# Two units of 576 and four of 720 tokens instead of seven of 576, with a six-place ring carried on from the first unit

## The reference

```python
k_p = k.reshape(B, H, Sp, 8, D).mean(axis=3)      # B = H = 8, D = 64, Sp = 576 // 8 = 72
v_p = v.reshape(B, H, Sp, 8, D).mean(axis=3)
attn = softmax(matmul(q, k_p.transpose(0, 1, 3, 2)) / sqrt(D))
x = matmul(attn, v_p).transpose(0, 2, 1, 3).reshape(4608, 512)
h = x @ moe_w_in;   g = s * relu(h) ** 2 + b;   x = g @ moe_w_out       # layer 0
h = x @ moe2_w_in;  g = h / (1 + exp(-h));      out = g @ moe2_w_out    # layer 1
```

## Time and profile before

| | us |
|---|---|
| three runs | 1695.22, 1687.95, 1694.45 (median 1694.45) |
| the profiled execution's own time | 1693.99 |
| its span, first to last instruction | 1692.2 |
| TensorE / DVE / ACT / GpSimd busy | 1614.3 / 1073.7 / 927.5 / 239.5 |
| mean granted TensorE clock | 0.982 of 2.4 GHz |
| DMA | 542.75 MB, mean 321 GB/s |

### The profile page before, as it was taken

The page is one execution under the profiler, slowest core; times in us unless marked ns, Lnnn a source line. Parts: engine busy times, 40 slices in busy tenths (PEclk is TensorE's granted clock), DMA queues, the critical chain, the costliest instruction groups (busy, mean ns, idle before and its releaser), DMA issues.

```text
span 1692.2 us, 29600 instructions
## 1 busy us (share of the span) xinstructions
PE 1614.3 (95%) x11926; PEld 1600.0 (95%) x11926; DVE 1073.7 (63%) x1309; ACT 927.5 (55%) x1286; POOL 239.5 (14%) x294
## 2 busy tenths in 40 slices
PE   7988997899999999999999999999999999999999
PEld 6988997899999999999999999999999999999998
DVE  6686677376574757557575674837657475654645
ACT  4574554565547555574555645556454755547443
POOL 5320220120201112011120201112011120000000
PEclk9999999999999999999999999999999999999999
DMA  6789787989898998989889898998989899899997
GB/s 191 278 321 346 297 313 291 394 295 326 300 374 306 340 322 301 378 307 332 303 317 376 298 339 306 359 350 299 325 295 384 307 333 316 272 391 330 331 327 259
DMA packets 155222, 542.75 MB, mean 321 GB/s; under 512 B 16592, under 2 KB 16592, under 8 KB 153040
## 3 DMA queue, kind: packets, MB, share of 16 engines
q1 hardware_dynamic: 150736, 531.43, 87.2%
q10 hardware_dynamic: 4352, 9.44, 1.4%
HBM read 464.39 MB, written 76.41 MB: 320 GB/s over the span
## 4 chain that ended last, share of the span: by engine, by line
PE 76%; DMA 10%; DVE 8%; ACT 3%; issue 2%; SPq 0%; DVEq 0%; ACTq 0%
PE a_ps L745 20%; PE a_ps L767 20%; PE b_ps L767 15%; PE b_ps L745 13%; DMA xa_dram<-probs 6%; PE a_ps L671 2%; DMA w_raw<-weights 2%; PE t_ps L625 2%; PE t_ps L638 2%; DMA ring<-w_dram 2%; DVE w_sum L1156 2%; DVE ring L1141 1%; PE t_ps L611 1%; ACT ring L840 1%; DVE gq L1200 1%
## 5 line engine op out<-in xcount | busy, mean ns | idle before, releaser
L745 PE MATMUL a_ps<-xc_hi,ring 128*128 128x288 f32 x1792 | 404.5, 304 | 20.2 <-DVE gq L1200 15.7
L767 PE MATMUL a_ps<-sp_hi,ring 128*128 128x288 f32 x1792 | 368.7, 295 | 1.4 <-DMA ring<-w_dram 1.4
L745 PEld LDWEIGHTS a_ps<-xc_hi,ring 128*128 128x128 f32 x1792 | 306.7, 193 | 24.0 <-DVE gq L1200 17.7
L745 PE MATMUL b_ps<-xc_hi,ring 128*128 128x288 f32 x1344 | 302.4, 300 | 13.7 <-DVE gq L1200 13.6
L767 PEld LDWEIGHTS a_ps<-sp_hi,ring 128*128 128x128 f32 x1792 | 291.2, 188 | 1.9 <-DMA ring<-w_dram 1.9
L1241 DVE TENSOR_TENSOR sp_lo<-gq,sp_hi 128x1152 fp32r<-128x1152 f32 (+1 forms) x182 | 198.1, 1101 | 132.5 <-ACT sp_hi L937 131.7
L767 PE MATMUL b_ps<-sp_hi,ring 128*128 128x288 f32 x1344 | 277.8, 295 | 0.6 <-DMA ring<-w_dram 0.6
L745 PE MATMUL a_ps<-xc_lo,ring 128*128 128x288 f32 x896 | 269.4, 301 | 0.0
L767 PE MATMUL a_ps<-sp_lo,ring 128*128 128x288 f32 x896 | 264.5, 295 | 0.0
L745 PEld LDWEIGHTS b_ps<-xc_hi,ring 128*128 128x128 f32 x1344 | 228.5, 191 | 15.3 <-DVE gq L1200 15.0
L937 ACT ACTIVATE sp_hi<-gq 128x1152 fp32r<-128x1152 f32 (+1 forms) x182 | 168.2, 940 | 126.5 <-PE b_ps L767 63.4
(11 more groups left out here) (168 smaller groups left out, 2570.6 us busy)
## 6 DMA issues: line engine op xcount, KB each, us to landing
ring<-w_dram SPq DMA_DIRECT2D x784, 512.0 KB, 5.6
w_dram<-w_stage SPq DMA_DIRECT2D x32, 1024.0 KB, 6.5
w_dram<-ring SPq DMA_DIRECT2D x48, 512.0 KB, 3.9
w_raw<-weights SPq DMA_DIRECT2D x16, 1024.0 KB, 6.4
out<-yb ACTq DMA_DIRECT2D x16, 576.0 KB, 7.2
k_stage<-kT SPq DMA_DIRECT2D x30, 288.0 KB, 5.7
q_sb<-qT SPq DMA_DIRECT2D x30, 288.0 KB, 6.0
v_stage<-vP SPq DMA_DIRECT2D x30, 288.0 KB
```

Source lines behind the costliest of these rows:

```text
L745: last = nc.tensor.matmul(bank[:, half, 0:th], w, xc_of(x, th)[:, j, k, :], start=(first and k == 0 and i == 0), stop=(k == 1 and i == 2), ...
L767: last = nc.tensor.matmul(bank[:, m, 0:th], w, split_of(g, th, turn, 2 * c + half), start=(first and half == 0 and i == 0), stop=(end and ...
```

## The change

Units have 576, 576, 720, 720, 720 and 720 tokens (`HALVES`). Attention stands six jobs beside each of units 0 and 1 (bases 2, 17, 32, 47, 62, 77), four beside each of units 2, 3 and 4 (0, 17, 56, 71), none beside unit 5; the first unit's third and fourth job begin at 66 and 83. The ring has six places, and granule n of unit 0 on goes to place (64 + n) mod 6, so that the first unit's granules and the next ones follow each other; the first four are asked for at i = 0, 1, 5, 6 of set 15. Split down pieces have four places (still written three pieces ahead). x is loaded into parts of `gq` that are free (behind its first unit's part, or where the third quarter ends), later in the odd phase (behind the low part of down piece 7), and ACT's first copy of an even phase waits until all of x is split. The raw weights, their sums and their stage lie over parts of `yb`, `xc_hi`, `xc_lo`, `sp_hi` and `sp_lo`. In the first unit the second half of a set's split stands at i = 6 instead of i = 2, its stores at 1, 2 and 7, DVE's `plain_out` first in its slot, and x is loaded behind slot 100 and used from 108.

```diff
-HALVES = (288,) * 7
+HALVES = (288,) * 2 + (360,) * 4
...
-XR_SLOTS = (11, 13, 15, 17, 19, 21, 23)
-RING = 8
+XR_SLOTS = (15, 17, 19, 21, 23, 25, 27)
+RING = 6
+PLACES = 4
...
-FIRST_XR = (36, 39, 42, 45, 48, 51, 54)
+LAST_LOADS = (0, 1, 5, 6)
+FIRST_XR = (44, 46, 49, 51, 54, 57, 59)
+XC_FIRST, SP_FIRST, G_FIRST = 14 * HB, 4 * PLACES * HB, 2 * FS * HB
...
+def place_of(n):
+    return (4 * SETS + n) % RING
...
-FIRST_TURNS = ((0, SPACED), (17, SPACED), (64, SPACED), (81, SPACED))
-TURN_SLOTS = ((0, SPACED), (17, OVER_EDGE), (SLOTS, TIGHT), (SLOTS + 15, TIGHT))
+FIRST_UP = 2
+FIRST_TURNS = ((0, SPACED), (17, SPACED), (66, SPACED), (83, SPACED))
+SIX = tuple((2 + 15 * n, TIGHT) for n in range(6))
+FOUR = ((0, SPACED), (17, OVER_EDGE), (SLOTS, TIGHT), (SLOTS + 15, TIGHT))
+UNIT_TURNS = (FIRST_TURNS, SIX, SIX, FOUR, FOUR, FOUR)
...
+        def x_of(ph):
+            s, layer = divmod(ph, 2)
+            if layer:
+                return yb[:, :]
+            at = 24 * HALVES[s - 1] if s else G_FIRST
+            return gq[:, at:at + 2 * KC * HALVES[s]]
...
+        def ring_stored(granule):
+            stored = [n for n in range(granule % RING, granule + 1, RING) if n % 4 != 2]
+            assert granule % 4 != 2
+            return r_stored[granule % RING], len(stored) * DMA
...
@@ load_gran
-                    sp.wait_ge(f_done, (SETS - 2 + n // 4) * PLAIN + PLAIN)
-                    if n % 4 != 2:
-                        sp.wait_ge(r_stored[n], SETS // 2 * DMA)
-                sp.dma_start(ring[:, n % RING, :].bitcast(F32), w_dram[row_of(ph, slot)]
+                    q, m = divmod(4 * SETS + n - RING, 4)
+                    sp.wait_ge(f_done, q * PLAIN + m + 5)
+                    sp.wait_ge(*ring_stored(4 * q + m if m != 2 else 4 * q + m - RING))
+                sp.dma_start(ring[:, place_of(n), :].bitcast(F32), w_dram[row_of(ph, slot)]
@@ load_x
-                    sp.wait_ge(xlo_ready, (2 * s - 1) * NPROD)
+                    sp.wait_ge(dlo_ready, (2 * s - 1) * SPLITS + PIECE_END[7])
@@ SP, first unit
-                if i < 4 and q + 1 < SETS:
-                    store_plain(q + 1, i)
+                if i in (1, 2, 7) and q + 1 < SETS:
+                    store_plain(q + 1, {1: 0, 2: 1, 7: 3}[i])
...
+                if q == SETS - 1 and i in LAST_LOADS:
+                    load_gran(0, LAST_LOADS.index(i))
...
-                if slot == FSLOTS - 30:
+                if slot == FSLOTS - 28:
                     load_x(0)
@@ SP, units
-                    if layer and slot == SLOTS_UP + RING + 3 and s + 1 < UNITS:
+                    if layer and slot == SLOTS_UP + RING + 10 and s + 1 < UNITS:
@@ ACT, prep_plain
-                if q >= 2:
-                    act.wait_ge(f_done, (q - 2) * PLAIN + 6 + 2 * n)
+                old_q, old_n = divmod(2 * q + n - RING // 2, 2)
+                if old_q >= 0:
+                    act.wait_ge(f_done, old_q * PLAIN + 6 + 2 * old_n)
@@ ACT, plain_out, layer 1
+                    act.wait_ge(f_sum, 4 * (SETS - 1))
+                    act.wait_ge(f_wlo, 2 * (SETS - 1))
@@ ACT, dhi
-                old_ph, old_idx = divmod(nth - 3, len(DOWN))
+                old_ph, old_idx = divmod(nth - PLACES, len(DOWN))
@@ ACT, part_up
+                if ph % 2 == 0 and g == 0 and j == 0:
+                    act.wait_ge(xlo_ready, (ph + 1) * NPROD)
@@ ACT and DVE, first unit
-                if i in (0, 2) and q + 1 < SETS:
-                    prep_plain(q + 1, i // 2)
+                if i in (0, 6) and q + 1 < SETS:
+                    prep_plain(q + 1, i // 6)
@@ DVE, first unit: the same two lines moved from the end of the slot to before prep_plain
                 if q % 8 == 7 and i % 2:
                     plain_out(q, i // 2)
```

More of the change, by code:

```diff
@@ L108 @@
 OVER_EDGE = (0, 1, 2, 3, 4, 6, 7, 8, 9, 11, 12, 14, 15)
-FIRST_TURNS = ((0, SPACED), (17, SPACED), (64, SPACED), (81, SPACED))
 TIGHT = (0, 1, 2, 3, 4, 6, 7, 8, 9, 11, 12, 13, 14)
-TURN_SLOTS = ((0, SPACED), (17, OVER_EDGE), (SLOTS, TIGHT), (SLOTS + 15, TIGHT))
+FIRST_UP = 2
[3 more added lines that the diff above has]
+UNIT_TURNS = (FIRST_TURNS, SIX, SIX, FOUR, FOUR, FOUR)
 def schedule():
     table, t = {}, PAIRS
[L117 to L121, removed]
+    for s, slots in enumerate(UNIT_TURNS, -1):
+        for base, offsets in slots:
             for i, name in zip(offsets, TURN_NAMES):
-                table[s, base + i] = (name, job)
-        t = upto
+                assert (s, base + i) not in table
+                table[s, base + i] = (name, t)
+            t += 1
+        assert t >= batches_for(s + 1) * PAIRS
     assert t == JOBS
@@ L217, in build, with over @@
         t_ps = psum("t_ps")
-        x_stage = probs[:, 0:S]
+        def over(name, at, columns, shape, dt=F32):
+            return nc.alloc_sbuf_tensor_at(name, [P] + shape, dt, offset=at + 4 * columns)
+        w_raw = [over("w_raw0", yb_at, 0, [4, 512]), sb("w_raw1", [P, 4, 512])]
+        w_sum = [over("w_sum0", xc_hi_at, XC_FIRST, [2, 512]), over("w_sum1", xc_lo_at, XC_FIRST, [2, 512])]
+        w_stage = [over("w_stage0", sp_hi_at, SP_FIRST, [2, GRAN], F32R), over("w_stage1", sp_lo_at, SP_FIRST, [2, GRAN], F32R)]
+        x_stage = probs[:, 0:S]
+        def x_of(ph):
[4 more added lines that the diff above has]
+            return gq[:, at:at + 2 * KC * HALVES[s]]
         def xc_of(buf, th):
@@ L449, in store_sum @@
                 sp.dma_start(w_dram[row:row + step + 1:step].rearrange("j p n -> p j n"),
-                             w_stage[:, (2 * q + n) % STAGE, :, :].bitcast(F32)).then_inc(done, DMA)
+                             w_stage[(2 * q + n) % STAGE][:, :, :].bitcast(F32)).then_inc(done, DMA)
             def sets_of(ph, slot):
@@ L684, in plain_down @@
                     if k == 3:
-                        pe.wait_ge(x_summed, 4 + 4 * layer)
+                        pe.wait_ge(x_summed, 2 * FIRST_UP * (1 + layer))
                     else:
@@ L751, in down @@
                 idx, c = divmod(slot - SLOTS_UP, 2)
-                (j, h), turn = DOWN[idx], (ph * len(DOWN) + idx) % 3
+                (j, h), turn = DOWN[idx], (ph * len(DOWN) + idx) % PLACES
                 n, th = gran(ph, slot) - 1, HALVES[ph // 2]
@@ L1144, in sum_set @@
             def sum_set(q, n):
-                a11, a12, a21, a22 = [w_raw[:, q % 2, i, :] for i in range(4)]
-                s1, s2 = w_sum[:, 0, :], w_sum[:, 1, :]
+                a11, a12, a21, a22 = [w_raw[q % 2][:, i, :] for i in range(4)]
+                s1, s2 = w_sum[0][:, 0, :], w_sum[0][:, 1, :]
                 if n == 0:
@@ L1155, in sum_set @@
                     left, right = ((s1, a11), (a12, s2), (a11, a21))[n - 1]
-                nc.vector.tensor_tensor(w_sum[:, n, :], left, right, ALU.subtract if n else ALU.add).then_inc(f_sum, 1)
+                nc.vector.tensor_tensor(w_sum[n // 2][:, n % 2, :], left, right, ALU.subtract if n else ALU.add).then_inc(f_sum, 1)
             def low_sum(q, n):
-                done = by_pair(w_stage[:, (2 * q + n) % STAGE, :, :])
+                done = by_pair(w_stage[(2 * q + n) % STAGE][:, :, :])
                 dve.wait_ge(f_whi, sum_split(q, n))
@@ L1350, in _ @@
                 attention(*turn_at(-1, slot))
-                if i in (0, 2) and q + 1 < SETS:
-                    prep_plain(q + 1, i // 2)
+                if q % 8 == 7 and i % 2:
+                    plain_out(q, i // 2)
+                if i in (0, 6) and q + 1 < SETS:
+                    prep_plain(q + 1, i // 6)
                 if i < 4:
@@ L1360, in _ @@
                     x_slot(0, XORDER[FIRST_XR.index(at)])
-                if q % 8 == 7 and i % 2:
-                    plain_out(q, i // 2)
             for ph in range(PHASES):
```

70 lines of the change are left out of this document (36 added, 34 removed).

## The result

The change makes the kernel 0.6% faster, a small gain but outside the interval of the noise: 1681.91 us median (1673.23 to 1686.48, 11 runs) against 1691.85 (1684.14 to 1698.28, 11 runs), ratio 0.9937, 95% interval 0.9912 to 0.9963. The prediction said 1650 with a range from 1608 to 1674: the sign is right, a gain of 42 was foretold and 10 came. The profiled execution took 1683.26 us, its span 1681.5.

What follows compares the result with a forecast made beforehand. It took TensorE's matmul stream and the holes in it as the bound. From 1692.2: matmul -17.5, attention's holes -8, first unit -8, gap -10.5, end +0.5 gave a 1648.7 span, forecast 1650 us, range 1608 to 1674.

Steps and rivals of the forecast that it cites:

- The additive 163.3 ns: Each 360-column matmul: a fixed 13.3 ns on top of its columns, 163.3 ns; the matmul term was -17.5 us.
- The proportional case: Rival on the 360-column matmul: cost grows with the columns, 166.3 to 166.6 ns, 18 us more, 1668; chance 0.24.
- the floor: Rival on the 360-column matmul: the extra is a floor, 152.3 to 156 ns, 1591 to 1611 us; chance 0.16.
- Attention's holes in the 720-token units: Units 2 to 4: six places where a job meets the store before it, 1.5 us each, 9 us.
- The first unit and the gap: First unit: the layer-edge hole and its low clock go, -8 us; gap before unit 0: PE goes straight on, -10.5 us.
- late next is a granule: Start of unit 0: last stores, y and ring loads meet, so a granule or ACT's part copy is late; 3 us given back.
- Attention's holes in units 0 and 1: Six jobs beside each unit leave 16 us of holes a unit, 32, plus 5 for ring loads over both.
- At 32 (down half, where pieces are split three ahead): 0.5: Units 0 and 1, job at slot 32: meeting the store of the job before it leaves a 0.5 us hole.
- Slot 54's hole: Units 0 and 1, job at 47: a low part behind DVE's slot 51 splits and sums comes some 4 us late.
- The ring starves units 0 and 1: Rival: six ring places starve units 0 and 1, slots of 2.0 us, 1735 us in all; chance 0.04.
- The holes don't shrink: Rival: 4.3 us at each of 16 places and 4 at both layer edges, 77 instead of 41, 1686; chance 0.06.
- Four split places: nothing: Four places for split down pieces change nothing, as the down halves run without a hole now.

Runs made afterwards that it cites:

- the first experiment: The changed kernel with seven units of 576 tokens again, four jobs beside each of the first six: 1683.8 us, ratio 0.9957 to the kernel before.
- the short sums: The changed kernel with five block sums in unit 0, and three sums and four low parts in unit 1, on 32 columns only: one run, span 1665.3 us.
- the own tile: The changed kernel with a separate tile for a job's finished x, so the next job's subtraction no longer waits for its store: 1666.0 us, ratio 0.9847.
- the moved jobs: The changed kernel with unit 0's six jobs at slots 2, 17, 38, 56, 71, 94 instead of 2, 17, 32, 47, 62, 77: 1667.07 us, ratio 0.9862.

## Why the prediction was wrong, step by step

**The sum, place by place**, profile against forecast:

| | forecast | measured |
|---|---|---|
| start of unit 0 (before 298.6) | 280.1 | 267.2 |
| units 0 and 1 | 436 | 479.7 |
| six 720-token layers with 12 jobs | 708 | 709.1 |
| the last unit and the end | 224 | 225.5 |

The forecast's column is its terms laid in order of time: 298.6 - 8 - 10.5; 4 x 89.4 + 12 jobs of 3.43 + 37; 6 x 109.6 + 41.2 + 9; 2 x 109.6 + 4.7 for the end. It sums to 1648, the measured one to 1681.5. The start was better by 13 us, two rows held within 2, and units 0 and 1 were 44 over, more than the whole miss. How much of the 13 is luck is open: with the same first unit, unit 0 starts at 271.9 in the profile of the first experiment, and at 264.3 in that of the short sums.

**The matmul: right.** The additive 163.3 ns is what the chain shows, 48 in 7.89 us and 24 in 3.94, 164 ns each:

```profile
1605.97 3.94 PE a_ps L784 x24
1621.73 3.95 PE a_ps L806 x24
...
1661.20 7.89 PE b_ps L806 x48
```

The layer is 110.4 us, not 109.6, and eight of them make it -11 over the kernel instead of -17.5: 1 ns a matmul, times 5376. The proportional case (166.3) and the floor (152) are out. The Trainium skill (TensorE: Matmul & The Clock Gate, Back-to-back issue gap) has N/2.4 + 2.5 ns as the warm gap of matmuls taken by themselves, and says that with weight loads between them both set the spacing. By the formula 360 columns take 152.5 ns; the trace disagrees, 164 here, as it did at 288. The floor of the forecast and this formula share only their value at 360 columns.

**Attention's holes in the 720-token units: right.** Forecast 9 us; 709.1 - 662.4 - 41.2 = 5.5, and the own tile took 5.7 away.

**The first unit and the gap: mechanism right, size low.** -16 for the first unit, where -8 was said (the bound was -12), and 12.7 for the gap, all of it, where 10.5 was; another 2.7 came from an earlier start. The 5.50 us wait at the layer edge is gone, and PE is idle for 6.7 us of the unit where it was for 19.0. But the 3 us set aside for "late next is a granule" were too few: PE stands 6.7 us for granules in the first slots (0.32, 1.52, 4.86), more than half of it by the y stores, as their removal shows (2.7 left). The forecast's sign of no ring wait above 3 us failed here (4.86) and, barely, at unit 0's load of x (3.02).

**Attention's holes in units 0 and 1: wrong.** The text gave "16 a unit" for the jobs and 5 for the ring, 37 in all. Measured: 479.7 - 357.6 - 41.2 = 80.9. The step that failed is the list of places where one job meets the store before it, and in it *"At 32 (down half, where pieces are split three ahead): 0.5"*. It took a buffer of pieces ahead as cover for PE's products and left out that the job's own turns have none: a transpose waits for a norm that stands in DVE's list behind splits and sums of 1.4 us each. The two even down halves hold 34 us of holes (with the lower clock behind them) where 9 were given (0.5 and 4 a unit); that is 25 of the 44 missed. Slot 54's hole, named in the forecast, came as told (3.58 us idle and the clock behind it). The rest of the miss is some 7 us at unit 0's start, 4 at the loads of x (9 instead of 5), and some 7 around slot 28 of the two odd layers, which no step named. There the transposes of a job's second turn wait (2.53 us before 460.42) for the low part of its first, and on DVE's timeline that stands behind two sums again (they end just before 459.61). No run shortened these sums, so that cause is read from the trace and not tried:

```profile
457.67 2.03 DVE L1269 TENSOR_TENSOR gq<-gq 128x576 f32<-128x576 f32 x2
459.61 0.75 DVE L1166 TENSOR_TENSOR pT_lo<-t_ps,pT_hi 72x576 fp32r<-72x576 f32 x1
```

The holes of the up halves were sized right (about 24 us against 23). That the even down half is the place, the moved jobs (-15), the short sums (4.30 to 1.17) and the own tile, which leaves these halves as long, show from three sides. What the three smaller holes of the half (1.52, 1.30, 1.17) hang on was not tried.

**Rivals.** "The ring starves units 0 and 1" was wrong as a mechanism: no slot was long all through. What six places cost comes once a load of x, some 3 us each, and more where there are more units: 20 us of median in seven units, the split places' part included. "The holes don't shrink" was right for units 0 and 1 and wrong for the rest. "Four split places: nothing" was right for the 720-token layers and wrong by 2 us in each crowded down half.

**Why a large change moved little.** By the two profiles, 10.7 us is what is left of three large parts. Unit 0 starts 31.4 earlier. Units 0 and 1 take 74.9 more (479.7, before 404.8 from 298.6 to 703.4), of which 13.7 are the work of four jobs moved there. All behind them takes 54.2 less, of which 13.7 are the same four jobs. The exchange of the units alone, with the own tile and a ring of eight, gives the same picture: -16 behind unit 1 and +45 in units 0 and 1. A ring of six costs a few us with wide units and up to 20 with narrow ones. The part that was not in the change, a tile of its own for x, is worth 16 with the wide units and 34 with seven narrow ones.

## What to carry to other kernels

Work moved into fewer, fuller stretches must be laid against the busiest engine's list there, slot by slot: a buffer ahead of the products covers the products, not the moved job's own chain. Before giving freed memory to a longer operand, price the reuse waits that it could end: here 2304 bytes a partition for one staging tile were worth more than the wider units. A prefetch ring should be sized by the worst moment of its queue (here the load of x), not by the median landing time.

## What the runs showed of the hardware

- One matmul of this kind is spaced at 133 ns with 288 columns and 164 with 360, at the higher clock level: 13 and 14 ns over the columns at 2.4 GHz. At 1.2 GHz, with 288 columns, nothing is over the earlier trace rows.
- A short hole costs more than its length. In unit 0's even down half PE is idle for 12.5 us (67.90 less 55.41), while the half is 16.5 longer than its work; the granted clock is 0.93 there:

```profile
332.00:399.90 67.90, 55.41 (x389) 53.90 (x389) 44.93 (x54) 26.91 (x34) 14.09 (x21) 0.93 0.80 268
```

- 512 KB loads landed in 4.5 us at the median; one took 12.20 when it was issued with two y stores (576 KB each) and the last 1 MB store of the sums under way, and its like 8.18 without the y stores.
